# One chip kernel of attention, routed experts and a feed-forward layer: a new order in the attention's tiles and in the routing tail, and all expert weights split in two parts

## What is computed

```python
# 1. attention, 2 batches x 8 heads x 576 positions x 64, sliding window of 128 with a distance bias
scores = q @ k.T / 8 - slope[h] * |i - j|      # only 0 <= i - j < 128
x = softmax(scores) @ v                        # then heads side by side: x is 1152 x 512
# 2. eight experts, one for each token, at most 288 tokens each
e = argmax(x @ w_gate); gate = softmax(x @ w_gate)[e]
slot = number of earlier tokens with the same e      # dropped if slot >= 288
y = gate * (relu(x @ w1[e]) @ w2[e])                 # w1: 512 x 1024, w2: 1024 x 512; 0 where dropped
# 3. feed-forward
h = y @ w_in; out = (h * sigmoid(h)) @ w_out         # 512 x 2048, 2048 x 512
```

## Time and profile before

| | us |
|---|---|
| Median of 3 runs | 486.25 (484.54 to 487.76) |
| The profiled execution's own time | 486.16 |
| Its span, first to last instruction | 484.4 |
| PE busy | 448.2, 93% of the span |
| Busy: DVE, ACT, POOL | 210.6, 209.1, 220.6 |
| First matmul of the experts | at 114.08 of the span |

### The profile page before, as it was taken

The page is one execution under the profiler, slowest core; times in us unless marked ns, Lnnn a source line. Parts: engine busy times, 40 slices in busy tenths (PEclk is TensorE's granted clock), DMA queues, the critical chain, the costliest instruction groups (busy, mean ns, idle before and its releaser), DMA issues.

```text
span 484.4 us, 8128 instructions
## 1 busy us (share of the span) xinstructions
PE 448.2 (93%) x2917; PEld 410.4 (85%) x2917; DVE 210.6 (43%) x659; ACT 209.1 (43%) x532; POOL 220.6 (46%) x162
## 2 busy tenths in 40 slices
PE   5898999825999999999999999999999999999993
PEld 4676777625999999999999989999999998999992
DVE  4677877652553644545545342222222222222220
ACT  4867677422554645446455544322222212222220
POOL 3006887756788878887686885200200001000002
PEclk9999999855999999999999999999999999999997
DMA  9999950119888988779975630000100000100001
GB/s 181 273 265 274 305 121 11 45 59 296 301 205 233 250 276 274 182 243 231 314 243 195 208 124 1 0 1 0 65 0 0 0 1 18 47 0 0 0 0 65
DMA packets 54422, 64.26 MB, mean 133 GB/s; under 512 B 31953, under 2 KB 31953, under 8 KB 54385
## 3 DMA queue, kind: packets, MB, share of 16 engines
q1 hardware_dynamic: 52608, 59.08, 43.0%
q0 software_dynamic: 1776, 4.73, 2.7%
HBM read 54.35 MB, written 9.44 MB: 132 GB/s over the span
## 4 chain that ended last, share of the span: by engine, by line
PE 81%; ACT 6%; SPq 4%; DMA 4%; DVE 2%; issue 1%; POOL 1%; POOLq 0%; DVEq 0%
PE bank L1080 14%; PE bank L1081 14%; PE bank L1082 13%; PE bank L1102 12%; PE bank L1138 9%; PE bank L1101 6%; PE bank L1099 4%; SPq L298 3%; ACT prob L530 3%; DMA q_raw<-in_q_dram 2%; PE bank L1100 2%; PE bank L994 2%; PE bank L1086 1%; PE bank L956 1%; DMA dispatched<-dispatch_dram 1%; PE bank L973 1%
## 5 line engine op out<-in xcount | busy, mean ns | idle before, releaser
L421 POOL TENSOR_TENSOR w_lo<-w_raw,w_hi 128x1024 fp32r<-128x1024 f32 x64 | 152.2, 2396 | 45.7 <-ACT w_hi L560 41.2
L912 DVE TENSOR_TENSOR g_full<-bank,sigmoid 128x384 f32<-128x384 f32 x48 | 26.8, 558 | 135.5 <-ACT sigmoid L640 135.3
L856 DVE TENSOR_REDUCE bank<-bank 128x192 f32<-128x384 f32 x96 | 54.3, 566 | 69.5 <-PE bank L1138 44.6
L501 POOL DMA_INDIRECT out_dram<-out_stage,permcol x9 | 8.8, 975 | 163.1 <-DVE out_stage L931 161.3
L640 ACT ACTIVATE sigmoid<-bank 128x384 f32<-128x384 f32 x48 | 23.6, 491 | 132.5 <-PE bank L1082 132.5
L1080 PE MATMUL bank<-x_hi,w_hi 128*128 x192 | 65.3, 340 | 0.0
L1082 PE MATMUL bank<-x_hi,w_lo 128*128 x192 | 64.7, 337 | 0.0
L1081 PE MATMUL bank<-x_lo,w_hi 128*128 x192 | 64.6, 336 | 0.0
L1102 PE MATMUL bank<-xT,w_hi 128*128 128x384 f32 x192 | 61.3, 366 | 0.0
L560 ACT ACTIVATE w_hi<-w_raw 128x1024 fp32r<-128x1024 f32 x58 | 60.9, 1050 | 0.0
L1080 PE MATMUL bank<-w_hi,g_hi 128*128 128x512 f32 x144 | 56.6, 393 | 0.7 <-DVE g_lo L916 0.7
(11 more groups left out here) (130 smaller groups left out, 788.7 us busy)
## 6 DMA issues: line engine op xcount, KB each, us to landing
w_raw<-in_moe_w_dram SPq DMA_DIRECT2D x64, 512.0 KB, 6.9
dispatched<-dispatch_dram SPq DMA_DIRECT2D x9, 576.0 KB, 8.6
dispatch_dram<-zeros SPq DMA_DIRECT2D x4, 1152.0 KB, 8.1
w_raw<-in_moe_w_in_dram SPq DMA_DIRECT2D x8, 512.0 KB, 4.6
w_raw<-in_moe_w_out_dram SPq DMA_DIRECT2D x8, 512.0 KB, 6.8
q_raw<-in_q_dram SPq DMA_DIRECT2D x8, 256.0 KB, 6.7
k_raw<-in_k_dram SPq DMA_DIRECT2D x8, 256.0 KB, 7.3
v_raw<-in_v_dram SPq DMA_DIRECT2D x8, 256.0 KB, 5.7
```

The costliest lines, as they stand in the source:

```text
L421: nc.gpsimd.tensor_tensor(wlo[s][:, sl], raw[s][:, sl], whi[s][:, sl], ALU.subtract).then_inc(pool_lo, 1)
L856: nc.vector.tensor_reduce(bk[:, 0:w], both, axis=AX.X, op=ALU.add).then_inc(summed, 1)
L912: nc.vector.tensor_tensor(gf[:, f % 2, :], bank[f % 4][:, 0:TB], sig[:, f % 2, :], ALU.mult).then_inc(gf_ready, 1)
```

## The change

1. **Order in a tile.** PE transposes the probabilities of half u - 1 before it takes up the output of tile t - 2; VectorE copies them before it normalizes and forms the logits' weights later.
2. **Routing tail.** Tile 9's values go to another PSUM bank (`out_bank`) and need not wait for tile 8's normalization; PE does the first half of them ahead of tile 8's logits. The rows in the table for tiles 8 and 9 are computed on VectorE (`slot_base`, `slot_found`) instead of GpSimd. ScalarE gates tiles 7, 8 and 9, each behind its own counters (`gate_x`), and the activation table for the sigmoid is loaded after expert 0.
3. **No fills.** The two fills of the experts' result (L468, L469) are gone from the narrow form; the wide form has them on VectorE.
4. **Rows in two loads.** `load_dispatched` loads two thirds (192 rows, all that the narrow form reads) and then the rest under its own counter. SP waits for the first part of expert 0's rows before it loads w1 of expert 1.
5. **All weights split.** `down` has eight split products. The eighth piece's low part is made by VectorE in step up 2; GpSimd makes seven. Pieces 6 and 7 of expert 0 get their high parts from ScalarE at the end of the tail. The down steps now wait for the low parts of all eight hidden chunks.
6. **Return order.** All ten `tell_places` go behind the last weight piece, and its load and the wait for it move to the end of the first feed-forward block.

```diff
-    SPLIT = 4
-    LOWS = SPLIT + 2 * KC
-    SPLITS = PIECES + PIECES * SPLIT // FC
+    LOWS = FC + 2 * KC
+    SPLITS = 2 * PIECES
+    EARLY = 6
+    POOLED = SPLITS - 1
...
+        def out_bank(t):
+
+            return bO if t < NTOK - 1 else bS[0][1]
...
             def load_dispatched(e):
-                sp.dma_start(xd[:], disp[bass.ds(e * C, C), :].rearrange("(s p) d -> p s d", p=SUB)).then_inc(xd_in, 16)
+                src = disp[bass.ds(e * C, C), :].rearrange("(s p) d -> p s d", p=SUB)
+                n = NARROW // SUB
+                sp.dma_start(xd[:, 0:n], src[:, 0:n]).then_inc(xd_in, 16)
+                if loaded[0] > 0:
+                    sp.wait_ge(xd_rest, 16 * loaded[0])
+                loaded[0] += 1
+                sp.dma_start(xd[:, n:], src[:, n:]).then_inc(xd_rest, 16)
...
             load_dispatched(0)
+            sp.wait_ge(xd_in, 16)
 
             sp.wait_ge(routed, 1)
...
             for t in range(NTOK):
                 r = ROWS[t]
-                slots(t)
-                if 1 <= t <= SPLITS:
+                if t < LAST:
+                    slots(t)
+                if 1 <= t <= EARLY:
                     high_here(t - 1)
 
                     pool.wait_ge(seen_ready, t + 2)
                     low_here((t - 1) // PIECES, (t - 1) % PIECES, t)
-                if t < NTOK - 2:
+                if t < LAST - 1:
                     pool.wait_ge(gate_ready, t + 1)
                     nc.gpsimd.tensor_scalar(xg[0:r, t, :], xt[0:r, t % 4, :], gate[0:r, t:t + 1], None, ALU.mult).then_inc(gated, 1)
                 pool.wait_ge(gated, t + 1)
                 if t == 0:
                     pool.wait_ge(zeroed, 16 * (NT - 1))
-                pool.wait_ge(slot_ready, t + 1)
+                if t < LAST:
+                    pool.wait_ge(slot_ready, t + 1)
+                else:
+                    pool.wait_ge(last_slots, t - LAST + 1)
                 nc.gpsimd.indirect_dma_start(disp, bass.IndirectOffsetOnAxis(sloti[0:r, t:t + 1], 0), xg[0:r, t, :], None,
                                              bounds_check=E * C - 1, oob_is_err=False).then_inc(scattered, 16)
-            pool.wait_ge(scattered, 16 * NTOK)
-            pool.wait_ge(routed, 1)
-            nc.gpsimd.memset(x2hi[:, :, C:].bitcast(F32), 0.0)
-            nc.gpsimd.memset(x2lo[:, :, C:].bitcast(F32), 0.0).then_inc(x2_zeroed, 1)
+            low_here(1, EARLY - PIECES, EARLY + 1)
...
             for e in range(1, E):
-                lows(e, 2 * (e % 2), range(SPLITS))
-                if e <= NTOK // 2:
-                    tell_places(2 * e - 2)
-                    tell_places(2 * e - 1)
+                lows(e, 2 * (e % 2), range(POOLED))
             lows(E, 0, range(2 * PIECES))
 
             for n in range(2 * PIECES):
                 low_here(2 + n // PIECES, n % PIECES, split_by(E, 2 * PIECES + n + 1))
+            for t in range(NTOK):
+                tell_places(t)
...
+            def gate_x(t):
+                r = ROWS[t]
+                act.wait_ge(gate_ready, t + 1)
+                act.wait_ge(x_ready, t + 1)
+                act.wait_ge(gated, t)
+                nc.scalar.activation(xg[0:r, t, :], xt[0:r, t % 4, :], ACT.Copy, scale=gate[0:r, t:t + 1]).then_inc(gated, 1)
+
             take_xT(NTOK - 2)
+            gate_exp(NTOK - 3)
             take_pT(U - 1)
+            gate_x(NTOK - 3)
             gate_exp(NTOK - 2)
             take_xT(NTOK - 1)
+            gate_x(NTOK - 2)
             gate_exp(NTOK - 1)
-
-            nc.scalar.activation(warm[:, 1, :], zeros[:, 0:E], ACT.Sigmoid)
-            act.wait_ge(gated, NTOK - 2)
-            for t in (NTOK - 2, NTOK - 1):
-                r = ROWS[t]
-                act.wait_ge(gate_ready, t + 1)
-                act.wait_ge(x_ready, t + 1)
-                nc.scalar.activation(xg[0:r, t, :], xt[0:r, t % 4, :], ACT.Copy, scale=gate[0:r, t:t + 1]).then_inc(gated, 1)
+            gate_x(NTOK - 1)
+            act.wait_ge(pool_lo, EARLY)
+            for p in range(EARLY, SPLITS):
+                weight_high(1, p - PIECES, 16)
...
-                        dst = hid[:, c, 0, 0:w] if c < SPLIT else hidf[:, c - SPLIT, 0:w]
-                        nc.scalar.activation(dst, bk[:, 0:w], ACT.Relu).then_inc(hi_ready, 1)
+                        nc.scalar.activation(hid[:, c, 0, 0:w], bk[:, 0:w], ACT.Relu).then_inc(hi_ready, 1)
...
+                    if e == 0:
+                        nc.scalar.activation(table[:], ident[:, 0:E], ACT.Sigmoid)
...
+            def slot_base(t):
+                r = ROWS[t]
+                start(nc.vector.tensor_scalar(sbase[0:r, t:t + 1], best[0:r, t:t + 1], -float(C), float(E * C), ALU.mult, ALU.add))
+
+            def slot_found(t):
+                r = ROWS[t]
+                at_t = slice(t, t + 1)
+                dve.wait_ge(places_read, t + 1)
+                link(nc.vector.tensor_scalar(sdrop[0:r, at_t], place[0:r, at_t], float(C), DROP, ALU.is_ge, ALU.mult))
+                nc.vector.scalar_tensor_tensor(sloti[0:r, at_t], sdrop[0:r, at_t], sbase[0:r, at_t], place[0:r, at_t],
+                                               ALU.add, ALU.add).then_inc(last_slots, 1)
...
-                if t >= 2:
-                    normalize(t - 2)
-                    logits_weigh(t - 2)
-                scores(u, 1)
                 if t >= 1:
                     take_pT(u - 1)
                 if t >= 2:
+                    normalize(t - 2)
+                scores(u, 1)
+                if t >= 2:
+                    logits_weigh(t - 2)
                     logits_sum(t - 2)
...
             place_found(NTOK - 3)
-            normalize(NTOK - 2)
+            gate_found(NTOK - 3)
             logits_weigh(NTOK - 2)
-            take_pT(U - 1)
             logits_sum(NTOK - 2)
             logits_min(NTOK - 2)
+            take_pT(U - 1)
             first_match(NTOK - 2)
+            slot_base(NTOK - 2)
+            normalize(NTOK - 2)
             sums_guarded(NTOK - 1)
             sums_inverted(NTOK - 1)
-            gate_found(NTOK - 3)
             place_found(NTOK - 2)
+            slot_found(NTOK - 2)
             gate_found(NTOK - 2)
             logits_weigh(NTOK - 1)
             logits_sum(NTOK - 1)
             logits_min(NTOK - 1)
             first_match(NTOK - 1)
+            slot_base(NTOK - 1)
             normalize(NTOK - 1)
+            gate_found(NTOK - 1)
             place_found(NTOK - 1)
-            gate_found(NTOK - 1)
+            slot_found(NTOK - 1)
...
-                        if (e, kind, c) == (0, "down", 0):
-                            dve.wait_ge(x2_zeroed, 1)
                         take_sum(bank[(KC + t) % 8], w)
+                    if (kind, c) == ("up", 2):
+                        s, sl = 2 * (e % 2) + 1, slice((PIECES - 1) * PIECE, PIECES * PIECE)
+                        dve.wait_ge(whi_ready, split_by(e, SPLITS))
+                        nc.vector.tensor_tensor(wlo[s][:, sl], raw[s][:, sl], whi[s][:, sl], ALU.subtract).then_inc(dve_lo, 1)
...
+                if s == 0 and 1 <= t < NTOK - 1:
 
                     pe.wait_ge(x_ready, t)
+                elif s == 0 and t >= 1:
+                    pe.wait_ge(scores_ready, QUAD * (U - 1))
...
+                if t >= 1:
+                    turn_p(u - 1)
                 if t >= 2:
                     turn_x(t - 2)
 
@@ -1034,7 +1085,6 @@
                         pe.wait_ge(places_read, t - 2)
                     logits(t - 2)
                 if t >= 1:
-                    turn_p(u - 1)
                     values(u - 2)
...
                     elif kind == "down":
-                        pe.wait_ge(hi_ready, hi_of(e, KC + c))
+                        pe.wait_ge(parts_ready, low_of(e, "up", KC + c))
...
                     else:
                         if c == 0:
-                            pe.wait_ge(pool_lo, split_by(e, SPLITS))
-                        for m in range(SPLIT):
+                            pe.wait_ge(pool_lo, pooled_by(e, POOLED))
+                            pe.wait_ge(dve_lo, e + 1)
+                        for m in range(FC):
                             if c == 0:
                                 pe.wait_ge(parts_ready, low_of(e, "up", m))
-                            product(bk, w, w2_of(whi[slot + 1], m, c), w2_of(wlo[slot + 1], m, c), hid[:, m], m == 0, False)
-                        for m in range(SPLIT, FC):
-                            if c == 0:
-                                pe.wait_ge(raw_in[slot + 1][m // 2], 16 * (e // 2) + 16)
-                                pe.wait_ge(hi_ready, hi_of(e, m))
-                            ins = nc.tensor.matmul(main_part(bk, w), w2_of(raw[slot + 1], m, c), hidf[:, m - SPLIT, 0:w],
-                                                   start=False, stop=(m == FC - 1))
+                            ins = product(bk, w, w2_of(whi[slot + 1], m, c), w2_of(wlo[slot + 1], m, c), hid[:, m], m == 0, m == FC - 1)
```

(16 more changed lines are left out.)

58 lines of the change are left out of this document (31 added, 27 removed).

## The result

The changed kernel takes **480.06 us** as the median of 4 runs (479.0 to 481.01), against 485.39 of the kernel before in the same set; the ratio is 0.9862 with a 95% interval of 0.9821 to 0.9903. Run again later beside the kernel before it gave 479.05 and 0.9857 (0.9825 to 0.9889). So it is faster, as forecast, by about 1.4%, but by less than half of the 12.5 that were forecast, and 480.06 lies above the range (470.5 to 479.0). The profiled execution takes 479.0, its span is 477.3; before, 486.16 and 484.4. That execution is 7.2 faster and ends on the upper bound of the range. In single executions of either kernel the clock falls in attention as well, for some microseconds or not at all; a time given as measured is the median of all executions and the ratios leave out the slowest of them, so kernels are compared by ratio, and stages by their own lengths.

What follows compares the result with a forecast made beforehand. The kernel was taken as bound by the chain through the routing tail and TensorE's work per expert: 486.16 - 4.6 (experts) - 5.9 (tail) - 2.0 (rows' load) = 473.7, with an 8-in-10 range of 470.5 to 479.

Steps and rivals of the forecast that it cites:

- Tail: Routing tail: new order and shorter chain land the last scatter at 102.2 instead of 108.15, -5.9 (bounds -4.5 and -7).
- the 0.8: Attention up to tile 9: scores of its second half 0.5 earlier, plus 0.3 from the tiles before 7.
- Rows in two loads: Load of expert 0's rows: smaller first part with w1 held back takes 3.9 instead of 5.86, -2.0.
- the experts' first matmul is then at 106.2: Start of the experts: TensorE's first matmul comes at 106.2 after tail and load savings, and a lap takes 19.05.
- the rest of 0.07: Chance 0.07 left for outcomes outside the forecast and named rivals, mostly small losses not seen.
- Down steps: Experts' down steps: splitting all products saves 0.16 a step, 5.1 over 32 steps, net -4.6.
- the walk: Low parts followed through a lap: the last is just in time at 11.8, 0.5 lost over eight laps.
- the first rival: Low parts late in the experts: the last comes 0.6 late, laps stay as long as before, 478.3; chance 0.15.
- w1 late: Start of the experts: late w1, or a rows' load as long as before, gives back 2 to 4; chance 0.12.
- shut out: VectorE gets in only after GpSimd's second piece: TensorE loses 2.4 a lap, 19 in all, 493; chance 0.04.
- Feed-forward: The stage after the experts was claimed untouched, with room for GpSimd's ten return-order scatters and one load.

Runs made afterwards that it cites:

- 7: Kernel of 2 with the old order within a block of tokens on TensorE and VectorE; 477.23, ratio 0.9805.
- Run 11: The changed kernel itself once more, unedited, on another chip beside the kernel before; 479.05, ratio 0.9857.
- 10: Kernel of 2 plus VectorE's weight piece in a down step, no SP hold on w1, 22 unread TensorE products before the first turn; 473.25, ratio 0.9731.
- 4: Changed kernel with SP asking for w1 of expert 1 only after VectorE's first low part; 481.75, ratio 0.9844.
- 5: Kernel of 2 without SP's wait for the rows before it asks for w1 of expert 1; 476.72, ratio 0.9776.
- 1: Changed kernel with GpSimd's last weight piece ahead of the experts waiting for VectorE's return order; 477.34, ratio 0.9781.
- 2: Changed kernel with VectorE branching right behind the offsets, return order behind the rows' low parts, w1 waiting for the offsets; 475.96, ratio 0.9735.
- 3: Changed kernel with the sides of VectorE's branch swapped, narrow form first; 480.01, ratio 0.9833.
- 9: Kernel before with only the split of all eight w2 pieces; 483.94, ratio 0.9937.
- 12: Kernel of 2 with GpSimd's ten scatters of places back between the laps of weight pieces; 477.42, ratio 0.9806.
- 8: Kernel of 2 with 20 unread TensorE products between the count and the first turn; 475.12, ratio 0.9763.

## Why the prediction was right, and where not

**Tail: right.** The rows were asked for at 103.16 (forecast 102.2), 5.0 earlier than before against 5.9 forecast. What is missing is attention: the order did bring its 0.6 in the last blocks before tile 9 (7), but in the profiled execution eight score products of the second block took 2.08 instead of 1.13; at the next scores it was 2.1 behind the kernel before, at tile 9 0.1. Run 11, without that stretch, reaches tile 9 at 86.13, 0.5 ahead. With the new order and a clock of 1.00 all through attention this place lies between 85.19 (10) and 87.39 (4) in six profiles, and the kernel before has one profile, so from the start to tile 9 the 0.8 is neither shown nor refuted. From there each step took what I gave it within 0.3: the logits at 95.20 (forecast 94.6), the slot ready at 99.57 (98.8), the scatter begun at 100.52 (99.7), all later by what attention didn't bring.

**Rows in two loads: right in size, wrong in cause.** 3.40 to the first turn instead of 5.91, -2.5 against -2.0; this half microsecond, which I did not foresee, is a part of why the profiled execution still ends on the bound of the range. The load itself took 3.4 where I took 3.9 by proportion, with w1 held back; the hold doesn't count (5). The row of 2.82 was as near. The fit of the Trainium skill, DMA: Bandwidth & Descriptors, Anatomy of one DMA, gave 2.9 as an estimate, about as far off on the other side; it is a fit of transfers that GpSimd issues, and this one is SyncE's.

**The step that failed: "the experts' first matmul is then at 106.2", and a lap from there.** I followed the chain that ended last and moved it forward by 7.9, and didn't ask whether VectorE, off that chain in the kernel before, would be ready 7.9 earlier. There it ended the return order at about 104.7, and TensorE's turn came at 114.08: 9.4 of slack that no row of the chain shows. The change took 7.5 of it and made VectorE itself later: GpSimd's weight piece, now behind the last scatter, lies upon `oo` (2.84 in the chain, 0.16 without it), so that the return order ends 1.2 later than before. Even the 9.4 flatter: the branch and the wait behind it took 5.0 in the changed kernel, so before, by this estimate, VectorE was ready at 109.7 for a first low part at 115.12, with 5.4 to spare. The change asks for 7.5 and 1.2 and is 3.3 short, which is TensorE's gap (3.29). This is the collision of the earlier trace rows, which I priced in the laps and not here; the Trainium skill, GPSIMD Engine Reference, 1. Specifications, states it for VectorE's instructions with two SBUF inputs, and `oo` is one. The branch's own 2.8 to 4.3 can't be seen before, since VectorE waits for the rows anyway; but the branch stood in the code. Together +3.2, shown by 1 (collision out: 2.3 of the gap gone), 2 (all gone) and 3 (the wait moves with the jump). In run 11, where the wait behind the jump is 2.83, the first lap is 14.99 instead of 16.00, so +2.2 and +3.2 are both this step. None of the rivals named it; it fell into the rest of 0.07.

**Down steps: the price right, the walk too tight.** A lap is 19.04 to 19.05 where the low parts are in time (forecast 19.05), and VectorE's own piece is 1.22 (1.1 to 1.5) and 2.96 beside GpSimd (3.0). I took 0.5 lost over eight laps, it was about 1.6, from these rows: 19.04 twice, once 19.62, then 19.25. The waits are where I said, for the low parts in the first down step (1.4 in total), so the first rival was right in kind at a third of its size. What I had wrong is that I counted the scatters of places only as load on GpSimd ("gone", a relief). They were the gap in which no weight piece of GpSimd stood beside VectorE's (9, 12). Each lap from expert 3 on loses 0.21 by their removal.

**w1 late, shut out: no.** w1 asked for at 106.53 held up nobody; VectorE always got in behind one piece.

**Feed-forward: not untouched.** Its one wait for `g_lo` grew from 0.72 to 1.08, all of the +0.4. It is GpSimd's piece beside the subtraction again, and no chance of one execution: it is 1.0 to 1.1 in every profile with all weights split, that of 9 included, except 3, where the jump stands there too.

What stays open: why the wait behind the jump is 2.83 in two profiles and 4.1 to 4.3 in two others, what sets off the slow stretches in attention, and why the clock fell again in 10 and not in 8.

## What to carry to other kernels

When a chain becomes shorter, list every engine that has to be ready at its end and when it is so now; the slack of the engines off the chain is the limit, and it isn't in the chain's rows. Put a branch over much code where its engine has nothing to do, as soon as its operand is known, and let the side that is taken follow directly. And before short DMA-issuing work is moved off a queue as pure load, look at what another engine does in that stretch.

## What the runs showed of the hardware

- Behind a taken jump over a long side of code VectorE executed nothing for 2.83 to 4.34. Behind the branch not taken its next instruction came after 1.65, released by ScalarE; the jump at the other end of the code then took 5.2 from one instruction to the next (3).
- VectorE's two-operand work beside a GpSimd piece: 1024 columns in 1.22 alone and 2.96 beside; a product of 80 columns in 0.24 and 2.9. The small one ends 0.1 behind GpSimd's piece (103.82), the big one 1.1: both pay the rest of the piece and then their own time. Beside GpSimd's issuing of a scatter the 1024 columns take 1.22 (9, 12).
- Twenty products that nobody reads brought the clock from 0.50 to 1.00 before the rows landed, at no cost to the chain (8). With 22 it was at 1.00 as well, and fell to 0.50 for 3.4 at the start of the experts, behind a wait of 1.75 (10).
